# Attention and two MLPs on one core: products of the first pairs in halves, loads and weight splits in another order

## The reference

```python
scores = (q @ k.T) / sqrt(64)                  # batch 2, 12 heads, 448 rows, head size 64
scores = cap * tanh(scores / cap)              # cap = 30
attn   = softmax(scores)                       # the reference subtracts the row maximum first
x      = attn @ v                              # gathered to 896 x 768
x      = relu(x @ w_in) ** 2 @ w_out           # 768 -> 2048 -> 768
out    = silu(x @ w_in2) @ w_out2              # 768 -> 2048 -> 768
```

## Time and profile before

| What | Value |
|---|---|
| three runs | 549.35, 551.14, 551.42 us, median 551.14 |
| profiled execution, its own time | 549.79 us |
| its span, first to last instruction | 547.9 us |
| PE busy | 535.4 us, 98% of the span |
| DVE, ACT, POOL busy | 376.1, 261.3, 82.1 us |
| attention, until the first MLP matmul | 96.1 us |
| granted TensorE clock, mean | 0.998 of full speed |
| DMA | 42.16 MB, 77 GB/s in the mean |

### The profile page before, as it was taken

How to read it: one execution, slowest core, us unless ns; L and a number is a source line. 1 busy time by engine, 2 the same in 40 slices (tenths; PEclk the granted TensorE clock), 3 DMA queues, 4 the chain that set the end, 5 groups by cost and what they waited for, 6 DMA issues and landing times.

```text
span 547.9 us, 7096 instructions
## 1 busy us (share of the span) xinstructions
PE 535.4 (98%) x2626; PEld 442.6 (81%) x2626; DVE 376.1 (69%) x597; ACT 261.3 (48%) x403; POOL 82.1 (15%) x54
## 2 busy tenths in 40 slices
PE   6999999999999999999999999999999999999995
PEld 5333333799999999999998999999999999999895
DVE  2199999977778652676799855556855345568985
ACT  3988889054444322454444434444533144454230
POOL 0999999300000000000000000000000000000000
PEclk9999999999999999999999999999999999999999
DMA  7888540151112201411122024202111141020645
GB/s 159 219 235 199 147 110 2 57 135 58 45 33 72 63 1 57 135 58 38 40 63 57 17 59 135 59 10 68 47 54 34 59 134 36 23 78 15 118 63 85
DMA packets 82116, 42.16 MB, mean 77 GB/s; under 512 B 26784, under 2 KB 79008, under 8 KB 82080
## 3 DMA queue, kind: packets, MB, share of 16 engines
q1 hardware_dynamic: 77952, 40.32, 28.6%
q10 hardware_dynamic: 4096, 1.38, 1.3%
q0 software_dynamic: 32, 0.00, 0.0%
HBM read 38.93 MB, written 2.75 MB: 76 GB/s over the span
## 4 chain that ended last, share of the span: by engine, by line
PE 76%; DVE 14%; issue 4%; SPq 3%; DMA 1%; ACT 1%; DVEq 0%; ACTq 0%
PE banks L494 25%; PE banks L496 25%; PE banks L495 25%; DVE den L815 3%; SPq L301 2%; DVE w_hl L866 1%; DVE x_hi L825 1%; DVE rinv L820 1%; DVE att_o L823 1%; DVE y L946 1%; DVE den_r L812 1%; DVE qk_f L800 1%; DMA qk_raw<-in_k_dram 1%; DVE qk_f L796 1%; SPq L322 1%
## 5 line engine op out<-in xcount | busy, mean ns | idle before, releaser
L494 PE MATMUL banks<-x_hi,w_hl 128*128 128x448 f32 x384 | 140.7, 367 | 0.0
L495 PE MATMUL banks<-x_lo,w_hl 128*128 128x448 f32 x384 | 140.5, 366 | 0.0
L496 PE MATMUL banks<-x_hi,w_hl 128*128 128x448 f32 x384 | 140.5, 366 | 0.0
L494 PE MATMUL banks<-g_hi,w_hl 128*128 128x448 f32 x336 | 123.3, 367 | 0.7 <-DVE w_hl L866 0.7
L496 PE MATMUL banks<-g_hi,w_hl 128*128 128x448 f32 x336 | 123.0, 366 | 0.0
L495 PE MATMUL banks<-g_lo,w_hl 128*128 128x448 f32 x336 | 123.0, 366 | 0.0
L494 PEld LDWEIGHTS banks<-x_hi,w_hl 128*128 128x128 f32 x384 | 72.1, 188 | 7.6 <-issue 1.4
L496 PEld LDWEIGHTS banks<-x_hi,w_hl 128*128 128x128 f32 x384 | 72.1, 188 | 6.2
L495 PEld LDWEIGHTS banks<-x_lo,w_hl 128*128 128x128 f32 x384 | 72.1, 188 | 6.2
L861 DVE TENSOR_TENSOR w_hl<-w_raw,w_hl 128x768 fp32r<-128x768 f32 x32 | 32.5, 1016 | 57.4 <-ACT w_hl L640 57.3
L494 PEld LDWEIGHTS banks<-g_hi,w_hl 128*128 128x128 f32 x336 | 63.1, 188 | 7.0 <-DVE w_hl L866 1.4
(11 more groups left out here) (64 smaller groups left out, 549.5 us busy)
## 6 DMA issues: line engine op xcount, KB each, us to landing
w_raw<-in_moe_w_in_dram SPq DMA_DIRECT2D x32, 384.0 KB, 3.4
w_raw<-in_moe_w_out_dram SPq DMA_DIRECT2D x24, 512.0 KB, 5.3
qk_raw<-in_k_dram SPq DMA_DIRECT2D x48, 112.0 KB, 2.7
qk_raw<-in_q_dram SPq DMA_DIRECT2D x40, 112.0 KB, 2.8
v_t<-in_v_dram SPq DMA_DIRECT2D x24, 96.0 KB, 2.8
out_dram<-rows SPq DMA_DIRECT2D x40, 56.0 KB, 2.2
qk_raw<-in_q_dram ACTq DMA_DIRECT2D x8, 112.0 KB, 4.1
out_dram<-rows ACTq DMA_DIRECT2D x8, 56.0 KB, 2.8
```

What stands on the lines that cost most here:

```text
L494: pe.matmul(dst, hi[:, kk, :], mov_hi, start=start, stop=False, skip_group_check=onto)
L495: pe.matmul(dst, hi[:, kk, :], mov_lo, start=False, stop=False, skip_group_check=onto)
L496: return pe.matmul(dst, lo[:, kk, :], mov_hi, start=False, stop=stop, skip_group_check=onto)
```

## The change

It has four parts.

- **PE, pairs 0 to 2.** `output` is cut in two: `output_first` (values of units 0 and 1, with the waits for `v_t`, `v_x` and the first exponentials) and `output_rest` (units 2 and 3). For the first pairs PE's list is written out: scores 0; first half of values 0; scores 1, units 0 to 2; rest of values 0; scores 1, unit 3; scores 2, unit 0; first half of values 1; scores 2, units 1 and 2; rest of values 1; scores 2, unit 3; denominators 0. From pair 3 on the loop is as before.
- **SP.** k of pair 2 is loaded ahead of part 0 of `v_x`, k and q of pair 3 ahead of part 1 of `v_t` and `v_x`.
- **ACT, weight tiles.** The first tile is cast after pair 7, the second after pair 9.
- **Group 1 of each stage, ACT and DVE.** In group 0 DVE makes all of `prod_low(1, 0)`, `w_s1`, `w_s3`, `w_s2` and `prod_low(1, 1)` right after `prod_low(0, 6)`, ahead of the additions to `y`; ACT casts the weights of product 1 of group 1 ahead of `x_high`.

```diff
--- before.py
+++ after.py
@@ -350,14 +350,18 @@
             sp.wait_ge(s_first_in[0], 4 * DMA)
             load_part(At(0, 1), 0, k_v, s_qk_in[1])
             load_v(0)
+            sp.wait_ge(s_turned, 2)
+            load_part(At(0, 2), 0, k_v, s_qk_in[0])
             load_v_x(0)
-            for j in range(2, PAIRS):
+            load_part(At(0, 2), 1, q_v, s_qk_in[0])
+            for j in range(3, PAIRS):
                 sp.wait_ge(s_turned, 2 * (j - 1))
                 load_qk(At(0, j))
-                if j % 2 == 0:
+                if j == 3:
+                    load_v(1)
+                    load_v_x(1)
+                elif j % 2 == 0:
                     load_v(j // 2)
-                if j == 2:
-                    load_v_x(1)
                 if j == 5:
                     for p in range(2):
                         load_w_in(0, 0, p)
@@ -459,7 +463,7 @@
                                      start=True, stop=True)
                 last.then_inc(s_att, 1)
 
-            def output(j):
+            def output_first(j):
                 if j.n in V_PARTS:
                     pe.wait_ge(s_v_in[V_PARTS.index(j.n)], 4 * DMA)
                 if j.n in V_PARTS[0:2]:
@@ -468,9 +472,15 @@
                 pe.wait_ge(s_exp, 2 * j.n + 1)
                 values(j, 0)
                 values(j, 1)
+
+            def output_rest(j):
                 pe.wait_ge(s_exp, 2 * j.n + 2)
                 values(j, 2)
                 values(j, CW).then_inc(s_val, 1)
+
+            def output(j):
+                output_first(j)
+                output_rest(j)
 
             pe.wait_ge(s_const, 1)
 
@@ -479,13 +489,22 @@
                     pe.matmul(ring[0][:, 0:P], warm_t[:, :], warm_t[:, :], start=True, stop=True)
             warm(WARM)
             pe.wait_ge(s_fill, 3)
-            for j in range(PAIRS):
+            for u in range(C):
+                scores(At(0, 0), u)
+            for j in range(2):
+                if j == 1:
+                    scores(At(0, 2), 0)
+                output_first(At(0, j))
+                for u in range(j, CW):
+                    scores(At(0, j + 1), u)
+                output_rest(At(0, j))
+                scores(At(0, j + 1), CW)
+            sums(At(0, 0))
+            for j in range(3, PAIRS):
                 for u in range(C):
                     scores(At(0, j), u)
-                if j > 1:
-                    sums(At(0, j - 2))
-                if j > 0:
-                    output(At(0, j - 1))
+                sums(At(0, j - 2))
+                output(At(0, j - 1))
             sums(At(0, PAIRS - 2))
 
             def passes(dst, w, kk, mov_hi, mov_lo, start, stop, onto=False):
@@ -655,8 +674,8 @@
             act.wait_ge(s_scale, 4)
             for j in range(PAIRS - 1):
                 weights(At(0, j))
-            for p in range(2):
-                tile_high(0, 0, p)
+                if j in (7, 9):
+                    tile_high(0, 0, (j - 7) // 2)
             weights(At(0, PAIRS - 1))
 
             def hidden_act(layer, s, p):
@@ -749,10 +768,14 @@
                             y_copy(layer, g, 1)
                         if g < GROUPS - 1:
                             prod_high(layer, s, g + 1, 0)
+                        if g == 0:
+                            prod_high(layer, s, 1, 1)
                         if x_too:
                             x_high(g, 0)
-                        if g < GROUPS - 1:
+                        if g == 1:
                             prod_high(layer, s, g + 1, 1)
+                        elif g == 0:
+                            pass
                         elif s == 0:
                             tile_high(layer, 1, 0)
                         elif layer == 0:
@@ -1113,29 +1136,33 @@
                         post_u3(layer, s, g)
                         prod_low(layer, s, g, 6)
                         if g == 0:
+                            prod_low(layer, s, 1, 0)
+                            w_s1(layer, s, 1)
+                            w_s3(layer, s, 1)
+                            w_s2(layer, s, 1)
+                            prod_low(layer, s, 1, 1)
                             if s == 1:
                                 post_12_u2(layer, g)
-                            w_s1(layer, s, g + 1)
                         post_22(layer, s, g)
                         if s == 1:
                             post_21_u3(layer, g)
 
-                        if not last:
+                        if g == 1:
                             prod_low(layer, s, g + 1, 0)
                         if s == 1:
                             post_11(layer, g)
                         leave(layer, s, g, 0)
-                        if not last:
+                        if g == 1:
                             w_s3(layer, s, g + 1)
 
                         if last and layer == 1 and s == 1:
                             leave(layer, s, g, 1)
-                        if not last:
+                        if g == 1:
                             w_s2(layer, s, g + 1)
                             prod_low(layer, s, g + 1, 1)
-                        elif s == 0:
+                        elif last and s == 0:
                             tile_low(layer, 1, 0)
-                        elif layer == 0:
+                        elif last and layer == 0:
                             tile_low(1, 0, 0)
                         post_12(layer, s, g)
             leave(1, 1, GROUPS - 1, 2)
```

## The result

The changed kernel took **556.37 us** (median of 6 runs, 555.72 to 557.89) where the kernel before took 550.62 (6 runs, 549.35 to 551.46): a ratio of 1.0111 [1.009, 1.0131], 5.75 us slower. I had forecast 555.2, in a range of 552.0 to 557.0. The profiled execution took 557.89 with a span of 556.1. It is the slowest of its six, 1.5 above the median, and the one of before (549.79) lies 0.8 under its own, so the two traces lie 8.1 us apart where the medians lie 5.75 apart. By the trace the forecast was 553.9, and the profiled execution took 4.0 us more.

A forecast was written before the change was run, and what follows sets the result against it. TensorE, busy for 98% of the span, with the POOL/DVE chain behind it, was taken as the bound. +3.8 (chain) + 1.5 (clock) - 1.2 (group 1) = +4.1 us on the median 551.14 gave 555.2, range 552.0 to 557.0.

The forecast's parts named there:

- the moved wait: Ahead of pair 1's scores, PE's first half of values 0 waits for v_x; gap grows from 2.97 to 5.5 us.
- the chain of POOL and DVE: POOL's adds of pair 2 wait for pair 0's later denominators, DVE follows, delay reaches the end in full: +3.8 us.
- the clock: In PE's 5.5 us gap before pair 0's values the granted clock falls to half: +1.5 us, between 0 and 2.0.
- Rivals C and D: Pair 0's values: C, halves fill the gap, 549.9 or 548.2, chance 0.05; D, moved wait hidden, 551.1, chance 0.05.
- T: Start of the first value matmul of pair 0, once v_x has landed: 17.5, from 16.7 to 18.3.
- PE from T on: PE's work through pair 3's scores ends at T + 14.2; pair 0's denominators start at T + 13.4, taking 0.97.
- waits for qk_f in pairs 4 to 11: Sign of a right forecast: PE, shifted +2.8 at pair 4's scores, waits for DVE's transposes from there on.
- Rival B: In attention only PE's own path counts, as DVE may slip past POOL: +0.9, 552.0, chance 0.12.
- rival A: The clock does not fall in PE's 5.5 us gap: +2.6, 553.7, chance 0.28.
- Casts: First weight tiles cast one at a time after pairs 7 and 9, covered by ACT's idle time: 0.
- Loads of pair 3: k and q of pair 3 come some 3.8 us earlier; PE's 0.2 us wait before pair 3's scores goes: 0.
- Group 1: Second stage of each MLP: earlier splits end late matmul starts, 0.6 lost twice: -1.2; next split just on time.

The follow-up runs named there:

- the last version: Kernel before with the moved loads, casts, group 1 with product 2's split moved too, and 13 zero matmuls in PE's gap, without the halves: 547.65 us.

## Why the prediction was right

The mechanism was the one forecast: the moved wait, the chain of POOL and DVE behind it, and the clock. The sizes were not, and they did not cancel. All of them erred the same way, and in the traces the loss is 8.1 us where the steps add up to 4.1. In the medians it is 5.75, 1.65 more than forecast. That the time came within 1.2 us of the 555.2 is in part luck: I added the sum to 551.14, the median of three runs, and that of six is 550.62. Rivals C and D needed T near 15 or earlier, and fall with the 18.60. By the steps, in the profiled execution:

1. *The moved wait.* T was 18.60 against 17.5 (16.7 to 18.3), so just outside its bounds. SP took 2.19 us for the four k DMAs, not 1.81, and 1.83 for the v_x ones, which had taken 2.21: the longer time went with the place in the queue, not with the load. So the last v_x DMA was issued at 14.6, past my 14.1 to 14.5. And it landed nearly 4 us later: I had taken the middle between 2.6 and 3.8, but the upper end held, as in the earlier trace rows. The figure of 2.0 us for the fixed part of a DMA, for the GpSimd path (the Trainium skill, DMA: Bandwidth & Descriptors, Anatomy of one DMA), gave an estimate of 16.1, 2.5 us too early; the trace speaks against using it for this load. The loads moved T by 2.0 us (16.58 with the halves alone).
2. *PE from T on.* Without the clock POOL's add came 14.69 us after T, where I had 14.4: right.
3. *The chain.* +8.03 at POOL's add, +8.05 at the denominators of pair 10: what POOL loses reaches the end in full. The run with only the denominators moved shows the same with 1.17 and 1.11. The distance to PE's own path was right too: +7.04 at the scores of pair 4, 1.0 less than the chain, as 2.8 was less than 3.8. The sign that I had given for it, waits for qk_f in pairs 4 to 11, is not in the list of waits: PE slips by about 0.1 us in every second pair, too little to be listed, and the rest is the 1.4 us wait for den_r. Rival B, PE's path alone, falls for the changed kernel. My reason for excluding it (`den` meets POOL's add in every pair) was too general: with the loads alone it does not.
4. *The clock.* It fell, so rival A falls. The price was 2.8 in the profiled execution and 2.1 between medians, against 1.5 (0 to 2.0). What failed is the way I bounded it: a stretch at half of 4.0 us, as at the start. The stretch was 10.2 us here and 3.4 to 6.8 in others, and only the part after T costs, when PE has work. Half of that part fits four traces (its bounds are read from the granted clock of short stretches): (24.3 - 18.6) / 2 = 2.85 here for 2.78 measured; (20.3 - 16.9) / 2 = 1.7 for 32.92 - 16.58 - 14.69 = 1.65 in the halves alone, where the clock fell only at 16.9; (21.1 - 15.6) / 2 = 2.75 for 32.93 - 15.58 - 14.69 = 2.66 with the wait moved; and (19.1 - 15.7) / 2 = 1.7 for 4.21 - 2.53 = 1.68 with the casts alone. The Trainium skill (TensorE: Matmul & The Clock Gate, Loop structure matters more than you think) has PE lose its clock in an idle wait of 8 us for a DMA; here 6.55 us did it. But the clock also fell behind a gap of 2.84 us in one trace and not behind one of 2.97 in another, of kernels that do the same up to there. So the length of a short gap did not decide it here, and a short gap was not safe.
5. *Casts:* 0, and 1.0006 alone. 6. *Loads of pair 3:* 0, and 1.0002 for the loads alone.
7. *Group 1.* -1.2 was forecast; it was 0.0 alone (0.9998), and +0.1 in the changed kernel's trace. The step that failed is "the next split ... is just on time": in the run of group 1 alone it was 0.24 us late, and the late starts took back 0.4 (changed kernel) to 0.5 us of the 1.2. The other 0.7 or 0.8 was lost to the slower start-to-start time, a term that the sum does not have. With the next split moved as well the median is 1.8 us lower (interval -2.4 to -0.8), which holds the -1.2; how much of it is the split and how much the start-to-start time was not separated.

Sum in the traces: 3.8 + 1.5 - 1.2 became 3.8 + 1.1 (T) + 0.3 (step 2) + 2.8 + 0.1 = 8.1. Of the 2.35 us between that and the medians' 5.75, 0.8 is the profiled execution of before lying below its median and 1.5 that of after lying above. Of the signs that I had named, the idle time of PE, the clock and the missing wait for w_hl came; T (18.60 for 16.7 to 18.3) and POOL's add (36.07 for 31 to 34) came later than named, and the waits for qk_f are not listed.

## What to carry to other kernels

Before a piece of work is moved into an engine's gap, read when *its* inputs land: on an in-order queue a filler that waits longer than the work behind it does not fill the gap but widens it. A wait belongs as late as the first instruction that reads the data; here that was worth 4.1 us. When a late producer is removed, look at once for the next one due, in numbers: "just on time" was 0.24 us late. And where a gain is under 1 us, compare how fast the same matmuls follow one another in the two traces, before the gain or its absence is put down to the edit.

## What the runs showed of the hardware

**Matmuls in the second halves of the stages start either 202.7 or 206.7 ns apart**, and keep to it for whole stretches. In the changed kernel (same columns as above):

```profile
168.00:218.00 50.00, 50.00 (x244) 1.00 0.13 37
...
389.00:439.00 50.00, 50.00 (x249) 1.00 0.14 37
```

The clock is 1.00 and the DMA share alike in both. Over the 252 matmuls of a second half that is 1.0 us: 51.86 against 50.87. It changes from one second half to the next, often at a late split, and once (near 296 us, with the wait for v_x moved) in the middle of one with no start more than 0.22 us after the last. In the first halves it is 204. What sets it was not found, and no run was made for it. The kernel before had one second half wholly at 206.7 and one partly, the changed kernel one wholly and two partly, the last version none; of its 2.5 us this is about 1.3, the rest are the late splits (0.6 each). The run with the denominators late had none wholly at 206.7, which is its 1.0 us. With the wait for v_x moved, the same instructions took 51.30 and 51.01 where the changed kernel's trace has 51.88 and 51.58.

**Some DVE operations wait out POOL's add.** `den`, 14 elements a partition, ends 0.03 to 0.05 us after an add of POOL in both phases. In the kernel before it starts at 35.67, behind the start of POOL's add of pair 3 (35.21 to 37.30), and ends at 37.33, after 1.66 us. With the loads alone it starts at 34.58, while POOL still has 0.57 us of the last add of pair 2 to do, and takes 0.62. There `x_lo` meets the next pair's adds and takes 2.38 us instead of 1.45. Which operation it is, is decided in the first pairs and then kept to the last. The Trainium skill (SBUF — State Buffer, Who interferes with whom) describes it as an exclusive lock on a shared port pair that the loser waits for; these rows agree.
